# Row means of a Fourier and two-layer kernel: one product per row on four column parts of the array

## The chip, the cores and the metric

One core of a Trainium2 chip. The metric is the device time of one execution in microseconds (us). The engines of the core are TensorE (PE in the profile, PEld its weight loads), VectorE (DVE), ScalarE (ACT), GpSimd (POOL) and SyncE (SP), which only issues transfers here. Transfers run on 16 DMA engines shared by all queues: SP's queue is the hardware queue (q1), GpSimd's accumulating transfers go through the software queue (q0).

## What is computed

```
X = fft(fft(x, axis=1), axis=2).real            # x: 2 x 3008 x 256
rms = sqrt(mean(X * X, axis=-1) + 1e-6)         # one mean per token, 6016 tokens
xn = X / rms * rms_g
h1 = silu(xn @ w_gate) * (xn @ w_val)           # 256 -> 1536
y1 = h1 @ w_out                                 # 1536 -> 256
h = y1 @ w_in                                   # 256 -> 2048
out = (h * cos(h)) @ w_out2                     # 2048 -> 256
```

The result is real and symmetric, so only half of the columns of the spectrum are made, and two mirrored tokens share one column.

## The kernel before

The first stage makes the spectrum. The sequence is split in 32 x 94; after a first transform `features(G)` and `sequence(G)` on TensorE make 34 rows of the grid (`G` = 0 to 33, 17 for each of the 2 batches), 94 columns each, in a loop over `G`. VectorE's `pq_copy` and ScalarE's `uv_copy` (two rows at a time, `p = G // 2`) move the results on, into `uv0` and `uv1`. In the same loop ScalarE, VectorE and GpSimd split the first weights (`w1`, `wo1`) into a high and a low part. The low parts of `w1` and `wo1` are completed by accumulating transfers that GpSimd issues (`w1_add`, `wo1_add`).

The means of squares go over partitions, so TensorE makes them. The 34 rows are cut into 9 parts of 3 to 5 rows (`PARTS`). For part `q`: ScalarE squares (`square`), GpSimd adds the two halves (`add_squares`), TensorE multiplies by one column of weights (`rms`, all rows of the part in one product of 282 to 470 columns into one PSUM partition), ScalarE copies this to `mean_row` (`mean_copy`, two buffers, so part `q` waits for `mean_in[q - 2]`), and SP spreads it to one partition per row (`spread_mean`). `RMS_AT` gives the `G` behind which the product of a part stands on TensorE, `MEAN_COPY_AT` the `p` of the copy. `root`, `recip` and `inverse` make 1 / rms from them, first for the six rows that the first tile needs, and SP stores it and loads it back over all partitions (`store_inv`, `load_inv`).

The second stage takes 6 tiles of 502 columns. In a tile `up1` makes gate and value for 12 chunks of 128, `down` multiplies them into the output of the first layer, two chunks behind; then `up2` and `down` do the same for 16 chunks of the second layer. Every product is done as three (`L518` to `L520`: high by high, high by low, low by high). Of each chunk VectorE forms gate and value, ScalarE takes Silu, GpSimd multiplies, ScalarE and VectorE or GpSimd make `h_hi` and `h_lo`.

Each engine runs its own instructions in the order in which they are written; semaphores tie them together. The queue of SP is written out by hand: in it stand, behind the loads of the inputs, the spreads of the nine parts, the stores of `uv0` and `uv1` to memory, the tile loads and the weight loads `wo1` (1.5 MB), `wo2` and `win2` (2 MB each, `wo_raw` and `win_raw` in the profile). `win2` is asked for when all six chunks of `w1_lo` have landed. In chunk 6 of the first tile ScalarE waits for `win2` and the last chunk of `wo1_lo` (`win2_part`). Two of the nine parts are late: their products stand in the first tile (`RMS_LATE`).

Of the kernel before, what the change touches and what calls it, by code (L numbers as in the profile page):

```python
# [37 lines left out]
MEANS = sum(len(p) for p in PARTS)  # L38
MAGIC = 1.5 * 2.0 ** 23
# [3 lines left out]
def tables():  # L43
# [5 lines left out]
    for b in range(2 * BATCH):  # L49
# [17 lines left out]
    const = np.zeros((P, 2))  # L67
    const[:, 0] = 2.0 / DIM
    const[0, 0] = 1.0 / DIM
    const[1:, 1] = 1.0  # L70
    f = lambda v, c: np.ascontiguousarray(v.reshape(v.shape[0], c), dtype=np.float32)
    return {"t_seq1": f(seq1, 2 * BATCH * 2 * K1), "t_feat": f(feat, FEAT + DIM),
            "t_seq2": f(seq2, K1 * N2), "t_const": f(const, 2)}


def build(nc, x, w1a, w1b, small, wo1, win2, wo2, t_seq1, t_feat, t_seq2, t_const, out):
    ctx = ExitStack()
    with ctx:
# [45 lines left out]
        mean_row = sb("mean_row", [ROWS, MEAN_COLS], o_i2h + WO1B)[0:1, :, :]  # L124
        assert 8 * SQUARES * MEAN_COLS <= WO2B and WO1B + 4 * ROWS * MEAN_COLS <= WI2B
# [30 lines left out]
        consts = sb("consts", [2], o_end + 2016)  # L156
# [5 lines left out]
        assert base + pad(o_end + 2304 + 16 * N2) + 4 * N <= 229344  # L162
        mean_w, mask = consts[:, 0:1], consts[:, 1:2]
# [67 lines left out]
        RMS_AT = [8, 9, 15, 21, 24, 28, 32]  # L231
        MEAN_COPY_AT = [2, 3, 7, 10, 11, 13, 15]
        RMS_LATE = range(len(RMS_AT), MEANS)

        def rms_bank(q):
            return 3 if q < len(RMS_AT) else 6 + q - len(RMS_AT)

# [22 lines left out]
        WO1_SPLIT_AT = {14: 0}  # L260
# [43 lines left out]
        def _(sp):  # L304
# [126 lines left out]
        def _(pe):  # L431
# [63 lines left out]
            def rms(q):  # L495

                a, z = part_cols(q)
# [76 lines left out]
            def tile(t, first=False):  # L574
# [13 lines left out]
                for i in range(2, C1):  # L588
                    up1(t, i, halves=(0,))
                    if first and i == 2:  # L590
                        rms(RMS_LATE[1])
                    up1(t, i, halves=(1,))
                    if first and i == 2:
                        pe.wait_ge(uv_main, LAST)
                        down(t, 0, tokens=(0,))
                        pe.wait_ge(mean_out, MEANS)
# [24 lines left out]
        def _(act):  # L621
# [40 lines left out]
            def square(q):  # L662
                a, z = part_cols(q)
                act.wait_ge(uv_main, part_end(q) + 1)
                if q >= SQUARES:
                    act.wait_ge(ms_done, q - SQUARES + 1)
# [5 lines left out]
            def mean_copy(q):  # L672
                a, z = part_cols(q)
                act.wait_ge(ms_done, q + 1)
                if q >= ROWS:
                    act.wait_ge(mean_in[q - ROWS], 16)
                nc.scalar.activation(mean_row[:, q % ROWS, 0:z - a], ps[0:1, rms_bank(q), 0:z - a],  # L677
                                     ACT.Copy, bias=EPS).then_inc(mean_out, 1)

            def root(group):  # L680
                rows = STAT_ROWS[group]
                for q in STAT_MEANS[group]:
                    act.wait_ge(mean_in[q], 16)
# [35 lines left out]
            for p in range(LAST // 2):  # L719
# [3 lines left out]
                if p == 13:  # L723
# [6 lines left out]
                split_step(p)  # L730

# [34 lines left out]
            def tile(t, first=False, last=False):  # L766
                for i in range(C1):
# [483 lines left out]
```

## Time and profile before

| | |
|---|---|
| Median of 3 runs | 987.53 us (987.35 to 987.87) |
| Profiled execution | 989.1 us |
| Its span | 987.1 us |
| Busy: TensorE, VectorE, ScalarE, GpSimd | 976.0, 743.3, 640.9, 349.5 us |
| First product of the second stage | 62.63 us |

The span is the part of the profiled execution that the instruction trace covers; times below are counted from its start. An idle time in brackets is that of the engine just before the row, with what ended it.

### The profile page before, as it was taken

How to read it: one execution, taken by the hardware profiler on the slowest of the kernel's cores; microseconds unless marked ns; L12 is line 12 of the kernel's file. 1: busy time of each engine (PE TensorE's matmuls, PEld its weight loads, DVE VectorE, ACT ScalarE, POOL GpSimd, SP SyncE). 2: the span in 40 equal slices, each digit the busy share in tenths (PEclk: the TensorE clock that was granted, in tenths of full speed). 3: DMA queues.
4: the chain of work that ended last, by engine and by line, in shares of the span. 5: the costliest groups of instructions: out<-in, count | busy, mean ns of one | idle time of the engine just before them, and what ended most of it. 6: DMA issues, size and time to landing. Idle time of an engine off the chain costs nothing.

```text
span 987.1 us, 12908 instructions
## 1 busy us (share of the span) xinstructions
PE 976.0 (99%) x4468; PEld 808.4 (82%) x4468; DVE 743.3 (75%) x1028; ACT 640.9 (65%) x801; POOL 349.5 (35%) x292
## 2 busy tenths in 40 slices
PE   8989999999999999999999999999999999999998
PEld 8868788888888888888888888888888888888886
DVE  6779878768877668877768887767887767887665
ACT  5578778774468775358775348776447876437777
POOL 0359776017640007650006751005761003771000
PEclk9999999999999999999999999999999999999999
DMA  9689202001010001010001010001000000100001
GB/s 328 170 202 258 61 1 53 1 1 43 1 42 2 0 1 42 0 32 10 0 0 42 0 32 11 0 0 42 0 29 3 0 0 0 42 0 0 0 0 42
DMA packets 14079, 36.77 MB, mean 37 GB/s; under 512 B 2616, under 2 KB 6680, under 8 KB 13656
## 3 DMA queue, kind: packets, MB, share of 16 engines
q1 hardware_dynamic: 11976, 31.62, 9.4%
q0 software_dynamic: 2064, 4.72, 2.7%
q8 instruction: 14, 0.23, 0.1%
q14 instruction: 25, 0.20, 0.1%
HBM read 22.33 MB, written 9.26 MB: 32 GB/s over the span
## 4 chain that ended last, share of the span: by engine, by line
PE 93%; DMA 2%; POOL 2%; DVE 2%; ACT 1%; issue 0%; SPq 0%; ACTq 0%; DVEq 0%
PE ps L518 30%; PE ps L519 30%; PE ps L520 30%; PE ps L474 2%; POOL work L1158 1%; DMA x_sb<-x 1%; DMA wo_lo<-wo_raw 1%; PE ps L492 1%; PE ps L490 1%; PE ps L504 1%; POOL h_lo L1069 0%; SPq L306 0%; DVE x_sb L857 0%; PE ps L460 0%; DVE uv_lo L906 0%
## 5 line engine op out<-in xcount | busy, mean ns | idle before, releaser
L518 PE MATMUL ps<-h_hi,wo_hi 128*128 128x502 f32 x672 | 261.5, 389 | 0.0
L520 PE MATMUL ps<-h_hi,wo_lo 128*128 128x502 f32 x672 | 261.5, 389 | 0.0
L519 PE MATMUL ps<-h_lo,wo_hi 128*128 128x502 f32 x672 | 261.4, 389 | 0.0
L1069 POOL TENSOR_TENSOR h_lo<-work,h_hi 128x502 fp32r<-128x502 f32 x92 | 101.8, 1114 | 372.9 <-ACT h_hi L753 369.9
L738 ACT ACTIVATE h_hi<-work 128x502 fp32r<-128x502 f32 x132 | 82.6, 626 | 173.9 <-POOL work L1158 173.8
L1056 DVE SCALAR_TENSOR_TENSOR work<-work,ps 128x1004 f32<-128x1004 f32 (+1 forms) x109 | 117.2, 1075 | 95.1 <-ACT work L835 94.7
L1042 DVE SCALAR_TENSOR_TENSOR work<-work,ps 128x1004 f32<-128x1004 f32 (+1 forms) x109 | 116.5, 1074 | 48.6 <-ACT work L821 48.5
L518 PE MATMUL ps<-x_hi,win_hi 128*128 128x502 f32 x384 | 150.0, 391 | 0.0
L519 PE MATMUL ps<-x_lo,win_hi 128*128 128x502 f32 x384 | 149.3, 389 | 0.0
L520 PE MATMUL ps<-x_hi,win_lo 128*128 128x502 f32 x384 | 149.2, 389 | 0.0
L518 PEld LDWEIGHTS ps<-h_hi,wo_hi 128*128 128x128 f32 x672 | 126.3, 188 | 26.7 <-DVE h_lo L959 0.6
L520 PEld LDWEIGHTS ps<-h_hi,wo_lo 128*128 128x128 f32 x672 | 126.3, 188 | 25.9
L519 PEld LDWEIGHTS ps<-h_lo,wo_hi 128*128 128x128 f32 x672 | 126.3, 188 | 25.7
L966 DVE SCALAR_TENSOR_TENSOR plus<-u,w,ps 128x502 f32<-128x502 f32 x144 | 105.8, 735 | 52.4 <-PE ps L520 51.7
L821 ACT ACTIVATE work<-ps 128x1004 f32<-128x1004 f32 (+1 forms) x109 | 98.2, 906 | 60.7 <-PE ps L520 59.9
L830 ACT ACTIVATE work<-work 128x1004 f32<-128x1004 f32 (+1 forms) x109 | 102.8, 943 | 31.1 <-DVE work L1042 30.3
L1158 POOL TENSOR_TENSOR work<-work,uv_t 128x502 f32<-128x502 f32 x72 | 99.1, 1399 | 47.0 <-DVE uv_t L975 45.0
L959 DVE TENSOR_TENSOR h_lo<-work,h_hi 128x502 fp32r<-128x502 f32 x172 | 114.2, 702 | 1.3
L518 PE MATMUL ps<-uv_hi,w_hi 128*128 128x502 f32 x288 | 112.7, 391 | 2.3 <-ACT mean_row L677 1.4
L520 PE MATMUL ps<-uv_hi,w_lo 128*128 128x502 f32 x288 | 111.9, 389 | 0.0
L519 PE MATMUL ps<-uv_lo,w_hi 128*128 128x502 f32 x288 | 111.9, 389 | 0.0
L753 ACT ACTIVATE h_hi<-work 128x1004 fp32r<-128x1004 f32 (+1 forms) x109 | 101.7, 938 | 14.6 <-PE ps L520 8.7
(87 smaller groups left out, 1282.0 us busy)
## 6 DMA issues: line engine op xcount, KB each, us to landing
out<-y_sb SPq DMA_DIRECT2D x10, 502.0 KB, 3.2
x_sb<-x SPq DMA_DIRECT2D x6, 768.0 KB, 10.8
w_lo<-w_f POOLq DMA_DIRECT2D x6, 512.0 KB, 7.6
uv_t<-uv_dram SPq DMA_DIRECT2D x6, 502.0 KB, 3.6
wo_raw<-wo SPq DMA_DIRECT2D x1, 2048.0 KB, 8.8
win_raw<-win SPq DMA_DIRECT2D x1, 2048.0 KB, 10.0
raw_b<-w1b SPq DMA_DIRECT2D x3, 512.0 KB, 12.8
raw_a<-w1a SPq DMA_DIRECT2D x3, 512.0 KB, 13.1
```

The lines of the kernel that those rows point to most:

```text
L518: nc.tensor.matmul(acc, w_hi, v_hi, start=start, stop=False)
L519: nc.tensor.matmul(acc, w_hi, v_lo, start=False, stop=False)
L520: return nc.tensor.matmul(acc, w_lo, v_hi, start=False, stop=stop)
L753: nc.scalar.activation(h_hi[j % 2][:, gs, 0:N], work[j % 4][:, gs, :], ACT.Copy).then_inc(hi_done, gs.stop - gs.start)
L821: nc.scalar.activation(work[j % 4][:, gs, :], ps[:, bank_pair(j) + gs.start:bank_pair(j) + gs.stop, 0:N], ACT.Copy, bias=MAGIC).then_inc(r ...
L830: nc.scalar.activation(work[j % 4][:, gs, :], work[j % 4][:, gs, :], ACT.Sin, scale=TURN / 2).then_inc(sin_done, gs.stop - gs.start)
L959: nc.vector.tensor_tensor(h_lo[j % 2][:, g, 0:N], work[j % 4][:, g, :], h_hi[j % 2][:, g, 0:N].bitcast(F32), ALU.subtract).then_inc(hid_sp ...
L966: nc.vector.scalar_tensor_tensor(out=plus[m][:, :], in0=u128[:, :], scalar=w128[:, m * C1 + i:m * C1 + i + 1], in1=ps[:, bank_pair(m), 0:N ...
L1042: nc.vector.scalar_tensor_tensor(out=buf, in0=buf, scalar=MAGIC, in1=pair, op0=ALU.subtract, op1=ALU.subtract).then_inc(frac_done, gs.stop ...
L1056: nc.vector.scalar_tensor_tensor(out=buf, in0=buf, scalar=1.0, in1=pair, op0=ALU.subtract, op1=ALU.mult).then_inc(cos_done, gs.stop - gs.s ...
L1069: nc.gpsimd.tensor_tensor(dst, src, hi.bitcast(F32), ALU.subtract).then_inc(s, 1)
L1158: nc.gpsimd.tensor_tensor(work[i % 3][:, g, :], work[i % 3][:, g, :], value[i % 2][:, g, :], ALU.mult).then_inc(h_done[g], 1)
```

## The change

Of a mean part each row gets a product of its own of 94 columns, with 32 equal columns of weights (`QUARTER` is 32), so that row `i` comes out on PSUM partitions 32 (i mod 4) to 32 (i mod 4) + 31; the fifth row of the last part goes to a second piece of columns ("round"). The constant grows from 2 to 33 columns. The copy then takes 94 columns of up to 128 partitions, and the spread reads one partition out of each 32. Besides this the order is changed in several places: product 3 and copy 3 one step earlier; the split of the scaled tile one step earlier; the last product and copy (part 8) from chunk 2 to chunk 3 of the first tile, in another bank; the copy of part 6 ahead of the first `wo1` split; on SP `store_inv` ahead of `load_tile`, `load_u128` behind `load_inv`, and the `wo1` load ahead of the spread of part 3; on GpSimd some sums moved; and one short Silu on ScalarE behind the first stage.

```
-    const = np.zeros((P, 2))
-    const[:, 0] = 2.0 / DIM
+    const = np.zeros((P, QUARTER + 1))
+    const[:, 0:QUARTER] = 2.0 / DIM
...
-        RMS_AT = [8, 9, 15, 21, 24, 28, 32]
-        MEAN_COPY_AT = [2, 3, 7, 10, 11, 13, 15]
+        RMS_AT = [8, 9, 15, 20, 24, 28, 32]
+        MEAN_COPY_AT = [2, 3, 7, 9, 11, 13, 15]
+        LAST_MEAN_AT = 3
...
-        WO1_SPLIT_AT = {14: 0}
+        WO1_SPLIT_AT = {15: 0}
...
             def spread_mean(q):
-                a, z = part_cols(q)
+                b, k = PART_ROWS[q]
                 sp.wait_ge(mean_out, q + 1)
-                sp.dma_start(stat[stat_rows(*PART_ROWS[q]), 0, :], mean_row[:, q % ROWS, 0:z - a]
-                             ).then_inc(mean_in[q], 16)
+                for r in range(rounds(q)):
+                    n = min(4, k.stop - k.start - 4 * r)
+                    sp.dma_start(stat[stat_rows(b, slice(k.start + 4 * r, k.start + 4 * r + n)), 0, :],
+                                 mean_row[0:QUARTER * (n - 1) + 1:QUARTER, q % ROWS, r * N2:(r + 1) * N2]
+                                 ).then_inc(mean_in[q], 16)
...
-            load_tile(0)
-            load_u128(0)
             sp.wait_ge(inv_done, 1)
             store_inv(0, (slice(0, 1), slice(1, FIRST_ROWS)), 0)
+            load_tile(0)
             sp.wait_ge(inv_out, INV_OUT[0])
             load_inv(0)
+            load_u128(0)
             spread_mean(2)
-            store_uv(0, (slice(FIRST_ROWS, K1 - 1), slice(K1 - 1, K1)))
-            spread_mean(3)
             sp.wait_ge(n1_done, 2 * NG)
             load(wo1_raw[:, :], wo1, wo1_in)
+            spread_mean(3)
+            store_uv(0, (slice(FIRST_ROWS, K1 - 1), slice(K1 - 1, K1)))
             spread_mean(4)
...
-                if q >= len(RMS_AT):
+                if q == RMS_LATE[0]:
                     pe.wait_ge(uv_main, LAST - 2)
-                nc.tensor.matmul(ps[0:1, rms_bank(q), 0:z - a], mean_w, squares[:, q % SQUARES, 0, 0:z - a],
-                                 start=True, stop=True).then_inc(ms_done, 1)
+                if q == RMS_LATE[1]:
+                    pe.wait_ge(plus_done, 2 * LAST_MEAN_AT + 2)
+                for i in range(rows):
+                    r, at = i // 4, i % 4 * QUARTER
+                    nc.tensor.matmul(ps[at:at + QUARTER, rms_bank(q), r * N2:(r + 1) * N2], mean_w,
+                                     squares[:, q % SQUARES, 0, i * N2:(i + 1) * N2], start=True, stop=True
+                                     ).then_inc(ms_done, 1)
...
                     up1(t, i, halves=(0,))
-                    if first and i == 2:
-                        rms(RMS_LATE[1])
+                    if first and i == LAST_MEAN_AT + 1:
+                        pe.wait_ge(mean_out, MEANS)
                     up1(t, i, halves=(1,))
...
+                    if first and i == LAST_MEAN_AT:
+                        rms(RMS_LATE[1])
...
-                if p == 13:
+                if p == 12:
                     split_uv(0)
...
+            act.wait_ge(recip_done, 1)
+            nc.scalar.activation(stat[0:1, 1, 0:1], stat[0:1, 1, 0:1], ACT.Silu)
...
-                        if first and i == 1:
-                            mean_copy(RMS_LATE[1])
...
+                    if first and i == LAST_MEAN_AT:
+                        mean_copy(RMS_LATE[1])
...
-                if G == 31:
+                if G == 30:
                     dve.wait_ge(uv_hi_done, 1)
                     lo_part(uv_lo[:, :, 0:N], uv_t[:, :, :], uv_hi[:, :, 0:N], uv_split)
...
             scale_uv(0)
+            scale_u128(0)
+            w1_add(2)
             add_squares(6)
-            w1_add(2)
-            scale_u128(0)
             w1_add(3)
+            add_squares(7)
             wo1_add(0)
-            add_squares(7)
```

The first place is SP's queue between the inverse of the first six rows and the spread of part 4. `stat<-mean_row` is the spread of a part, here of parts 2 and 3, `wo_raw<-wo 128x3072` the load of `wo1`, `uv_dram<-uv` the store of batch 0. Before:

```order
L363 DMA u_90<-uv_dram 128x502
L343 DMA inv_dram<-stat 1x48 [waits inv_done]
L343 DMA inv_dram<-stat 5x94
L359 DMA inv_t<-inv_dram 128x502 [waits inv_out]
L334 DMA stat<-mean_row 4x1x94 [waits mean_out]
L351 DMA uv_dram<-uv_83 128x2x940 [waits uv_main]
L351 DMA uv_dram<-uv_83 128x2x48
L334 DMA stat<-mean_row 4x1x94 [waits mean_out]
L306 DMA wo_raw<-wo 128x3072 [waits n1_done]
```

And in the changed kernel:

```order
L360 DMA inv_dram<-stat 1x48 [waits inv_done,pq_done,uv_stored]
L360 DMA inv_dram<-stat 5x94
L372 DMA uv_t<-uv_dram 128x2x502
L376 DMA inv_t<-inv_dram 128x502 [waits inv_out]
L380 DMA u_90<-uv_dram 128x502
L350 DMA stat<-mean_row 4x94 [waits mean_out]
L320 DMA wo_raw<-wo 128x3072 [waits n1_done]
L350 DMA stat<-mean_row 4x94 [waits mean_out]
L368 DMA uv_dram<-uv_83 128x2x940 [waits uv_main]
L368 DMA uv_dram<-uv_83 128x2x48
```

The spread of part 3 (the second `stat<-mean_row`) stood ahead of the `wo1` load and now stands behind it.

The second place is ScalarE in the first tile. `work<-work` with `g_ready` is the Silu of a chunk, `mean_row<-ps` the copy of a mean part. Before, from the Silu of chunk 0:

```order
L779 ACTIVATE work_74<-work_74 128x1004 [waits g_ready]
L669 ACTIVATE squares<-uv_84 128x940 [waits ms_done,uv_main]
L677 ACTIVATE mean_row<-ps 1x376 [waits mean_in5,ms_done]
L738 ACTIVATE h_hi_78<-work_74 128x502 [waits h_done1,uv_stored]
L738 ACTIVATE h_hi_78<-work_74 128x502 [waits h_done0]
L677 ACTIVATE mean_row<-ps 1x470 [waits mean_in6,ms_done]
L779 ACTIVATE work_75<-work_75 128x1004 [waits g_ready]
```

In the changed kernel, from the Silu of chunk 3:

```order
L805 ACTIVATE work_74<-work_74 128x1004 [waits g_ready]
L726 ACTIVATE wo_hi<-wo_raw 128x1024
L728 ACTIVATE wo_lo<-wo_hi 128x1024 [waits wo1_hi_done]
L702 ACTIVATE mean_row<-ps 128x94 [waits mean_in6,ms_done]
L702 ACTIVATE mean_row<-ps 32x94
L766 ACTIVATE h_hi_79<-work_74 128x502 [waits h_done1,down_done]
```

The copy of part 8 moved from ahead of the second Silu to behind the fourth and its two split copies. SP issues the 2 MB load of `wo2` behind the spread of this part in both kernels:

```order
L350 DMA stat<-mean_row 4x94 [waits mean_out,uv_stored]
L350 DMA stat<-mean_row 4x94 [waits mean_out] x3
L350 DMA stat<-mean_row 1x2x47
L320 DMA wo_raw<-wo 128x4096 [waits uv_done]
L368 DMA uv_dram<-uv_84 128x2x48 [waits uv_main]
```

This is SP's queue of the changed kernel; before, the row `1x2x47` was part of one transfer of five rows.

## Rows read from the trace of the kernel before

**Rows 1.** The page, part 1: busy time and share of each engine.

```profile
PE 976.0 (99%) x4468; PEld 808.4 (82%) x4468; DVE 743.3 (75%) x1028; ACT 640.9 (65%) x801; POOL 349.5 (35%) x292
```

**Rows 2.** Timeline of TensorE, first stage: start, duration, what.

```profile
40.03 0.61 PE L474 MATMUL ps<-feat,g_sb 128*96 128x129 f32 x4
...
41.70 0.68 PE L474 MATMUL ps<-feat,g_sb 128*96 128x129 f32 x4
...
42.42 0.39 PE L492 MATMUL ps<-seq,pq 96*128 96x94 f32 x2
42.64 0.61 PE L474 MATMUL ps<-feat,g_sb 128*96 128x129 f32 x4
...
43.50 0.61 PE L474 MATMUL ps<-feat,g_sb 128*96 128x129 f32 x4
...
59.78 0.79 PE L504 MATMUL ps<-squares,consts 128*1 128x376 f32 x2
```

**Rows 3.** Timeline of TensorE, its stops and two chunk starts.

```profile
51.68 0.64 PE L504 MATMUL ps<-squares,consts 128*1 128x282 f32 x2 [1.09 <-ACT mean_row L677]
...
62.63 0.47 PE L518 MATMUL ps<-uv_hi,w_hi 128*128 128x502 f32 x1 [0.57 <-DVE uv_lo L906]
...
66.44 0.49 PE L518 MATMUL ps<-uv_hi,w_hi 128*128 128x502 f32 x1 [1.35 <-ACT mean_row L677]
...
73.95 0.95 PE L504 MATMUL ps<-squares,consts 128*1 128x470 f32 x2 [0.79 <-issue]
...
79.02 0.39 PE L518 MATMUL ps<-uv_hi,w_hi 128*128 128x502 f32 x1
...
84.46 0.39 PE L518 MATMUL ps<-uv_hi,w_hi 128*128 128x502 f32 x1
...
114.48 0.49 PE L518 MATMUL ps<-uv_hi,w_hi 128*128 128x502 f32 x1 [0.37 <-DVE uv_t L975]
```

**Rows 4.** Timeline of ScalarE in the first tile, and the chain that ended last.

```profile
74.94 0.55 ACT L677 ACTIVATE mean_row<-ps 1x470 f32<-1x470 f32 x1 [1.40 <-PE ps L504]
...
86.41 1.06 ACT L702 ACTIVATE wo_lo<-wo_hi 128x1024 fp32r<-128x1024 f32 x1
...
105.39 1.16 ACT L707 ACTIVATE win_hi<-win_raw 128x512 fp32r<-128x512 f32 x2 [3.83 <-DMA wo_lo<-wo_raw]
...
94.11 11.20 DMA wo_lo<-wo_raw
```

**Rows 5.** Timeline of SP's queue: issues of the spread of part 2 and two loads.

```profile
49.57 1.13 SPq L334 DMA_DIRECT2D stat<-mean_row  x1
...
76.27 0.43 SPq L306 DMA_DIRECT2D wo_raw<-wo  x1
...
94.06 0.35 SPq L306 DMA_DIRECT2D win_raw<-win  x1
```

**Rows 6.** Transfers by issue, 50 to 56 and 76 to 80 us: size, median us to landing.

```profile
wo_raw<-wo SPq DMA_DIRECT2D x1, 1536.0 KB, 10.2
...
wo_raw<-wo SPq DMA_DIRECT2D x1, 2048.0 KB, 8.8
...
uv_dram<-uv SPq DMA_DIRECT2D x2, 48.0 KB, 12.0
```

**Rows 7.** Stretches: busy time of each engine, granted clock, DMA share, GB/s.

```profile
62.50:66.00 3.50, 2.46 (x14) 2.10 (x14) 2.05 (x5) 2.45 (x4) 0.04 (x1) 1.00 1.11 196
78.00:105.30 27.30, 27.30 (x122) 22.64 (x121) 23.90 (x39) 20.34 (x26) 23.26 (x20) 1.00 0.96 279
79.00:82.00 3.00, 3.00 (x15) 2.48 (x14) 2.84 (x5) 2.82 (x4) 3.00 (x4) 1.00 1.00 410
```

**Rows 8.** Timeline of VectorE's weight mixing and GpSimd's product beside it.

```profile
54.23 1.43 DVE L927 SCALAR_TENSOR_TENSOR w_f<-raw_a,gvec,raw_b 128x512 f32<-128x512 f32 x1
...
53.86 2.73 POOL L1115 TENSOR_TENSOR uv_t<-uv_t,inv_t 128x502 f32<-128x502 f32 x2 [1.67 <-DMA inv_t<-inv_dram]
...
75.34 0.74 DVE L927 SCALAR_TENSOR_TENSOR w_f<-raw_a,sm,raw_b 128x512 f32<-128x512 f32 x1
```

More of the change, by code:

```diff
@@ L38 @@
 MEANS = sum(len(p) for p in PARTS)
+QUARTER = P // 4
 MAGIC = 1.5 * 2.0 ** 23
@@ L123, in build @@
         squares = sb("squares", [SQUARES, 2, MEAN_COLS], o_o2h)
-        mean_row = sb("mean_row", [ROWS, MEAN_COLS], o_i2h + WO1B)[0:1, :, :]
-        assert 8 * SQUARES * MEAN_COLS <= WO2B and WO1B + 4 * ROWS * MEAN_COLS <= WI2B
+        ROUNDS = (max(max(p) for p in PARTS) + 3) // 4
+        mean_row = sb("mean_row", [ROWS, ROUNDS * N2], o_i2h + WO1B)
+        assert 8 * SQUARES * MEAN_COLS <= WO2B and WO1B + 4 * ROWS * ROUNDS * N2 <= WI2B
         feat = sb("feat", [FEAT + DIM], o_o2l)
@@ L161, in build @@
         inv_t = sb("inv_t", [N], pad(o_end + 2304 + 16 * N2))
-        assert base + pad(o_end + 2304 + 16 * N2) + 4 * N <= 229344
-        mean_w, mask = consts[:, 0:1], consts[:, 1:2]
+        o_const = pad(o_end + 2304 + 16 * N2) + pad(4 * N)
+        consts = sb("consts", [QUARTER + 1], o_const)
+        assert base + o_const + 4 * (QUARTER + 1) <= 229344
+        mean_w, mask = consts[:, 0:QUARTER], consts[:, QUARTER:QUARTER + 1]
         ga, gb, g128 = sm[:, 0:1], sm[:, 1:2], sm[:, 2:3]
@@ L229, in part_end, with rounds, mean_rows, quarters @@
             return b * STEPS + k.stop - 1
-        RMS_AT = [8, 9, 15, 21, 24, 28, 32]
-        MEAN_COPY_AT = [2, 3, 7, 10, 11, 13, 15]
+        RMS_AT = [8, 9, 15, 20, 24, 28, 32]
+        MEAN_COPY_AT = [2, 3, 7, 9, 11, 13, 15]
         RMS_LATE = range(len(RMS_AT), MEANS)
+        LAST_MEAN_AT = 3
+        assert len(RMS_LATE) == 2
         def rms_bank(q):
-            return 3 if q < len(RMS_AT) else 6 + q - len(RMS_AT)
+            return 3 if q < len(RMS_AT) else 6 if q < MEANS - 1 else bank_pair(1)
+        def rounds(q):
+            return (PART_ROWS[q][1].stop - PART_ROWS[q][1].start + 3) // 4
+        def mean_rows(q):
+            return sum(k.stop - k.start for _, k in PART_ROWS[:q + 1])
+        def quarters(q):
+            return min(4, PART_ROWS[q][1].stop - PART_ROWS[q][1].start) * QUARTER
         def parts_ending(p):
@@ L495, in rms @@
             def rms(q):
-                a, z = part_cols(q)
+                rows = PART_ROWS[q][1].stop - PART_ROWS[q][1].start
                 pe.wait_ge(const_in, 16)
@@ L595, in tile @@
                         down(t, 0, tokens=(0,))
-                        pe.wait_ge(mean_out, MEANS)
+                        pe.wait_ge(mean_out, MEANS - 1)
                         down(t, 0, tokens=(1,))
@@ L665, in square @@
                 if q >= SQUARES:
-                    act.wait_ge(ms_done, q - SQUARES + 1)
+                    act.wait_ge(ms_done, mean_rows(q - SQUARES))
                 if q == 0:
@@ L672, in mean_copy @@
             def mean_copy(q):
-                a, z = part_cols(q)
-                act.wait_ge(ms_done, q + 1)
+                act.wait_ge(ms_done, mean_rows(q))
                 if q >= ROWS:
-                    act.wait_ge(mean_in[q - ROWS], 16)
-                nc.scalar.activation(mean_row[:, q % ROWS, 0:z - a], ps[0:1, rms_bank(q), 0:z - a],
-                                     ACT.Copy, bias=EPS).then_inc(mean_out, 1)
+                    act.wait_ge(mean_in[q - ROWS], 16 * rounds(q - ROWS))
+                for r in range(rounds(q)):
+                    z = quarters(q) if r == 0 else QUARTER
+                    last = nc.scalar.activation(mean_row[0:z, q % ROWS, r * N2:(r + 1) * N2],
+                                                ps[0:z, rms_bank(q), r * N2:(r + 1) * N2], ACT.Copy, bias=EPS)
+                last.then_inc(mean_out, 1)
             def root(group):
@@ L682, in root @@
                 for q in STAT_MEANS[group]:
-                    act.wait_ge(mean_in[q], 16)
+                    act.wait_ge(mean_in[q], 16 * rounds(q))
                 nc.scalar.activation(stat[rows, 1, :], stat[rows, 0, :], ACT.Sqrt).then_inc(root_done, 1)
@@ L1159, in tile @@
                                                 value[i % 2][:, g, :], ALU.mult).then_inc(h_done[g], 1)
-                    if first and i == 0:
-                        add_squares(MEANS - 1)
                     if i == C1 - 2:
@@ L1164, in tile @@
                     lo1(t, i, 1, hid_ready_first)
+                    if first and i == 0:
+                        add_squares(MEANS - 1)
                     if first and i in W1_SPLIT_LATE:
```

7 lines of the change are left out of this document (3 added, 4 removed).

## Prediction

> **What bounds the kernel now.** I read the page first: TensorE is busy 99% of the span [rows 1], so a stage counts only through the stops of TensorE and through what it computes there. Then I read TensorE in order of time. In the first stage it goes round a loop over 34 columns of the grid, one every 0.86 us (from 42.64 to 43.50), and a mean product makes one step 1.67 (40.03 to 41.70) and the next 0.94 [rows 2]. All stops after the loads lie between 50 and 115 us [rows 3]: 1.09 us at 51.68 for a mean row's copy, 0.57 at 62.63 for `uv_lo`, 1.35 at 66.44 for the seventh mean row, 0.79 at 73.95 for the last mean product, and 0.37 at 114.48. From there no wait of TensorE is listed to the end of the span, and 24 products of 502 columns take 5.44 us (79.02 to 84.46), 0.227 each.
>
> The stop of 0.37 us looks like nothing, but it is the one that decides. ScalarE stands still for 3.83 us until 105.39 for the transfer that `win2_part` waits for, and the chain that ended last goes through that landing: issued 94.11, 11.20 us, landed 105.31 [rows 4]. From there it runs through the copies of `win_hi`, `h_hi` of chunk 6, VectorE's chunk 8 and to TensorE at 114.48. So there is next to no slack behind the landing: if it comes later, TensorE waits later by the same amount, and nothing behind it is idle that could take the loss up. What sets the landing is bandwidth: the 16 DMA engines are busy 0.96 of the 27.3 us from 78.00 to 105.30 [rows 7]. That stretch begins when SP issues the 2 MB load of `wo_raw` at 76.27 [rows 5], and SP issues it behind the spread of the last mean row, which ScalarE finished at 74.94 + 0.55 = 75.49 [rows 4].
>
> **The change part by part.**
>
> *The last mean (part 8).* Before, its product stands in chunk 2 of the first tile, its copy before ScalarE's second Silu. Now the product stands behind `down` of chunk 1 (that is, in chunk 3), and the copy behind Silu and both copies of `split_wo1` in chunk 3. At the old pace chunk 3 ends on TensorE at 84.46 [rows 3]; behind the Silu of chunk 3 the `wo_lo` copy starts at 86.41 and ends 1.06 later, at 87.47 [rows 4]; two copies of 94 columns are estimated at 0.5 together, since one of 470 columns takes 0.55. So at an unchanged pace the last mean row is out at 88.0 instead of 75.49.
>
> SP takes its queue in order: spread of part 8 (now two transfers), `wo_raw` 2 MB, the store of batch 1, `win_raw`. From the mean row to the issue of `wo_raw` SP took 0.78 (75.49 to 76.27); one more issue adds about 0.65. From the issue to the busy stretch it is 1.73 (76.27 to 78.00), and then come 27.3 us of transfers, less what can now run earlier. That is the two accumulations of chunks 4 and 5 into `w_lo`, which hang on GpSimd and not on SP: 1.05 MB, at the 196 GB/s of a stretch with such accumulations [rows 7] 5.3 us. The rest, `wo_raw`, the store, `win_raw` and two accumulations into `wo_lo`, is 22.0 us. The win load itself may be asked for earlier than 94.06 [rows 5], but it queues behind 3.5 MB of the same queue. That a later transfer of one queue doesn't overtake is seen in the 48 KB stores issued behind the 2 MB load: they land after 12.0 us, the load after 8.8 [rows 6].
>
> So the landing is (last mean row) + 0.78 + 0.65 + 1.73 + 22.0 = last mean row + 25.2.
>
> *When the last mean row comes.* Four things move it from 88.0.
> Earlier: the `rms(3)` product and its copy move one step forward, which should remove the 1.09 at 51.68; `store_inv` stands ahead of the two loads, `uv_hi` and `uv_lo` are made one step earlier, which takes away the 0.57; the seventh mean is copied before the split of `wo1`, which takes away the 1.35; and the last mean product with its wait leaves chunk 2 (0.79 and the 0.9 that it takes). Together at most 4.7 us.
> Later, first: the load of `wo1` (1.5 MB) now stands ahead of the spread of part 3. It took 10.2 us to land [rows 6]; issued behind the spread that stood at 49.57 [rows 5], and somewhat sooner, beside an accumulation, it ends near 59 to 61, and the spread of part 3 behind it no sooner. The copy of part 5 reuses that row's buffer (`mean_in3`), and `rms(6)` waits for the copy. TensorE reached that product at 59.78 before [rows 2], and less the 1.09 plus six parts of dearer products it is there at about 59.8 again, so I take a new stop of 1.5 us, between 0 and 2.5 (ScalarE's copy can't be done before 60, and its own start takes time).
> Later, second: the row products. One of 94 columns in this loop takes 0.22 (42.42 to 42.64) [rows 2], four take 0.88. A product of 376 columns adds 0.81 + 0.08 = 0.89 to the loop, its start and end included. The new form isn't in the trace: below, it costs nothing more or saves what two passes overlap; above, 0.3 more per part. I take 0.2, for seven parts 1.4, nearest to the rows of 94 columns.
> Later, third: VectorE and GpSimd. The mixing of weights took 1.43 on VectorE at 54.23, while GpSimd multiplied from 53.86, and 0.74 at 75.34, when GpSimd was idle [rows 8]. Now the second Silu no longer waits for the last mean, so GpSimd's product of chunk 1 falls on the two late mixes. Two of them cost up to 2 x 0.7 us more; I take 1.4 (0 to 1.7), and the up product of chunk 3 waits for VectorE behind them.
> Sum: 88.0 - 4.7 + 1.5 + 1.4 + 1.4 = 87.6; ScalarE is busy in this stretch and takes up part of any difference, so I use 87.3, with 82.5 and 89.5 as ends.
>
> *The release.* 87.3 + 25.2 = 112.5, against 105.3: 7.2 later. TensorE's own work is near its old place there (the four terms cancel within 1 us), so it stops for about 7 us in chunk 8, first at `down` of chunk 6, whose `h_hi` is behind the waiting `win2_part` on ScalarE.
>
> *What costs nothing.* The copies of the other mean rows (fewer columns each than before) lie on ScalarE, which waits elsewhere. The constant of 33 columns instead of 2 is 17 KB under the first loads. The Silu table loaded before the wait (1.3 us) helps only where ScalarE is late in chunk 0; it isn't. Without that cover each would be worth under 1.5 us.
>
> **A page beside the rows.** The row shows 0.22 us for each 94-column product, and nothing of four that overlap [rows 2]. The Trainium skill, "TensorEngine Tiling (Array Packing)", Key Properties, says that tiles of the array run independently and in parallel, and that a change of tiling mode drains the engine. By it four row products would take little more than one, some 0.6 less a part, by the rows 1.4 more in all. The sum to the release hardly moves by this, since the stop for `mean_in3` takes up what TensorE gains before it; the last mean row would come about 1 us sooner.
>
> **The sum.** The profiled execution took 989.1 us for a span of 987.1, the median of the runs is 987.53. Plus 7.2: span 994.3, profiled 996.3, median 994.7.
>
> **The rivals.**
> *Transfers run faster* (ends on the other side). In the stretch from 79 to 82 they moved 410 GB/s, against 279 over the whole [rows 7]. With the accumulations out of the way, the remaining 6.6 MB could go at 410: 16 us instead of 22. With the last mean row at 87.3 the release is at 106.5, 1.2 later: 988.7, no change. If the row comes at 83.3 (all the 4.7 kept) the release is at 102.5 and TensorE keeps up to 2.5: 985.0. The point from which it is a gain is a last mean row before 84. Against it: stretches with stores and accumulations never came near 410, and they make up half of what is left.
> *The first stage gains all and the transfers stay*: 83.3 + 25.2 = 108.5, plus 3.2: 990.7. This is slower too, only smaller.
> *The long stop lowers TensorE's clock.* No row of this trace has TensorE idle for more than 1.5 us after the loads, and the granted clock is 1.00 in every stretch listed [rows 7]; a stop of 7 us is outside what it shows. At half the clock, 1.2 in place of 2.4 GHz, a 502-column product takes about twice its 0.227; over some 12 products that is 2.7 us: 997.4. The Trainium skill, "TensorE: Matmul & The Clock Gate", Part 1, says that an idle engine falls back to 1.2 GHz. This makes the loss larger than the sum.
> *The change does nothing*: if the loads of batch 1 and `wo2` didn't hang on the last mean, the moves inside the first stage would cancel: 987.5. SP's order speaks against it.
>
> **How the numbers follow.** Within 0.2% (985.6 to 989.5) is about what a measurement of this kernel can't tell from no change. The forecast (992 to 996.5) has 0.56, the clock rival (above 996.5) 0.14, the smaller loss (989.5 to 992) 0.14, no change 0.08, faster 0.08. The range from 989 to 999.5 leaves out the faster cases, most of no change, and a stop with a longer clock loss. Slower 0.84, same 0.08, faster 0.08.
>
> **What would show it.** Right: SP issues the 2 MB `wo_raw` load near 88 to 89 us and not 76; the DMA engines stand nearly idle from about 78 to 88; ScalarE's wait for `win_raw` or `wo_lo` is about 8 to 12 us instead of 3.8 and ends near 112; TensorE has one stop of 5 to 8 us near 113 to 119 and none of size behind it; a stop for a mean row near 59 to 61. Wrong: the last mean row out before 84; DMA at over 350 GB/s from its issue on; the landing under 106; or a loss that lies at the means themselves.

## The result, and the profile after

The changed kernel takes 994.54 us (median of 5 runs, 992.32 to 996.86) against 987.87 (5 runs beside it): ratio 1.0059, 95% interval 1.0035 to 1.0084. Forecast: 994.7 (989.0 to 999.5). The profiled execution took 996.86 us, span 995.0 (before 989.1 and 987.1). A second profile, taken later of the same kernel, took 993.09 us, span 991.2; the two differ in one place that matters below, so both are shown.

The page (part 1 answers to [rows 1]; part 6, issues to landing, to [rows 6]):

```profile
PE 978.2 (98%) x4518; PEld 813.3 (82%) x4518; DVE 743.5 (75%) x1028; ACT 639.0 (64%) x803; POOL 351.2 (35%) x292
...
wo_raw<-wo SPq DMA_DIRECT2D x1, 2048.0 KB, 9.6
win_raw<-win SPq DMA_DIRECT2D x1, 2048.0 KB, 19.6
```

The chain over the last mean row: timeline of ScalarE, then of SP's queue, first profile (answers to [rows 4, 5]):

```profile
57.75 0.25 ACT L702 ACTIVATE mean_row<-ps 128x94 f32<-128x94 f32 x1 [1.26 <-DMA stat<-mean_row]
...
87.98 0.35 ACT L702 ACTIVATE mean_row<-ps 128x94 f32<-128x94 f32 x2
...
112.42 1.15 ACT L733 ACTIVATE win_hi<-win_raw 128x512 fp32r<-128x512 f32 x2 [8.20 <-DMA win_raw<-win]
...
89.56 0.40 SPq L320 DMA_DIRECT2D wo_raw<-wo  x1
...
92.81 0.37 SPq L320 DMA_DIRECT2D win_raw<-win  x1
```

The last row is out at 87.98 + 0.35 = 88.33, SP issues the 2 MB load of `wo2` 1.23 us later, and 22.8 us after that `win_raw` has landed and ScalarE goes on. The waiting instruction is the same as before; it ends 7.0 us later.

TensorE, same profile (answers to [rows 2, 3]): two row-product places, the stop at part 6, and the stop at the release with the pace behind it:

```profile
40.22 0.37 PE L525 MATMUL ps<-squares,consts 128*32 128x94 f32 x8
40.52 0.68 PE L491 MATMUL ps<-feat,g_sb 128*96 128x129 f32 x4
...
58.14 0.52 PE L525 MATMUL ps<-squares,consts 128*32 128x94 f32 x8 [1.75 <-ACT mean_row L702]
58.59 1.18 PE L491 MATMUL ps<-feat,g_sb 128*96 128x129 f32 x4
...
88.38 0.49 PE L540 MATMUL ps<-uv_hi,w_hi 128*128 128x502 f32 x1 [1.17 <-ACT mean_row L702]
...
115.82 0.49 PE L540 MATMUL ps<-h_hi,wo_hi 128*128 128x502 f32 x1 [4.04 <-DVE h_lo L979]
...
116.90 0.62 PE L540 MATMUL ps<-h_hi,wo_hi 128*128 128x502 f32 x1
117.32 0.62 PE L541 MATMUL ps<-h_lo,wo_hi 128*128 128x502 f32 x1
```

Stretches of it (columns as in [rows 7]):

```profile
62.50:66.00 3.50, 3.50 (x16) 3.10 (x15) 1.87 (x3) 2.12 (x3) 0.89 (x1) 0.64 0.79 144
70.00:78.00 8.00, 6.23 (x25) 3.91 (x23) 7.97 (x9) 5.44 (x7) 8.00 (x7) 1.00 0.00 0
...
90.00:112.40 22.40, 21.78 (x97) 17.64 (x95) 15.54 (x24) 10.43 (x13) 11.95 (x11) 1.00 0.93 304
...
114.00:118.00 4.00, 2.18 (x6) 1.79 (x7) 3.28 (x4) 4.00 (x7) 3.48 (x3) 0.78 0.01 2
```

The DMA engines stand still from 70 to 78, and from 78 to 88 their share is 0.40; before, the 2 MB load was issued at 76.27 [rows 5]. TensorE's granted clock, 1.00 all through the kernel before, is mixed with the lower level (1.2 GHz) in two places: behind the stop at 58.14 and behind the stop of 4.04 us at 115.82, where products start 0.42 us apart instead of 0.227.

In the second profile only the second drop is there (timelines of TensorE and ScalarE):

```profile
58.04 0.37 PE L525 MATMUL ps<-squares,consts 128*32 128x94 f32 x8 [1.25 <-POOL squares L1124]
...
83.85 0.35 ACT L702 ACTIVATE mean_row<-ps 128x94 f32<-128x94 f32 x2
...
108.08 1.15 ACT L733 ACTIVATE win_hi<-win_raw 128x512 fp32r<-128x512 f32 x2 [7.99 <-DMA win_raw<-win]
...
111.48 0.79 PE L540 MATMUL ps<-h_hi,wo_hi 128*128 128x502 f32 x1 [3.83 <-DVE h_lo L979]
```

The two profiles start the product of part 6 on TensorE within 0.1 us of each other; from there the first falls 4.1 us behind (last row 88.33 against 84.20), and its release, the point at which ScalarE goes on, comes at 112.42 against 108.08. In that stretch lie some 6.5 us at the lower clock, from 58.6 to 65.2.

### The profile page after: what moved, and what is told of

The parts are those of the page before. It is cut to its first block, busy times and chain, and to the rows that moved or that the text cites. A ratio compares the mean times of both kernels' runs of the same rounds, so it can differ in the third digit from the quotient of the medians.

```text
span 995.0 us, 13011 instructions
## 1 busy us (share of the span) xinstructions
PE 978.2 (98%) x4518; PEld 813.3 (82%) x4518; DVE 743.5 (75%) x1028; ACT 639.0 (64%) x803; POOL 351.2 (35%) x292
## 4 chain that ended last, share of the span: by engine, by line
PE 91%; DMA 4%; DVE 2%; SPq 1%; POOL 1%; issue 0%; ACT 0%; DVEq 0%; ACTq 0%; POOLq 0%
PE ps L540 30%; PE ps L542 29%; PE ps L541 29%; DMA win_raw<-win 2%; PE ps L491 1%; DMA x_sb<-x 1%; DMA stat<-mean_row 1%; PE ps L509 1%; PE ps L507 1%; POOL work L1186 0%; SPq L320 0%; DVE plus L994 0%; DVE w_f L955 0%; DVE x_sb L885 0%; PE ps L477 0%
## 5 line engine op out<-in xcount | busy, mean ns | idle before, releaser
L766 ACT ACTIVATE h_hi<-work 128x502 fp32r<-128x502 f32 x132 | 82.5, 626 | 176.9 <-POOL work L1186 176.7
L987 DVE TENSOR_TENSOR h_lo<-work,h_hi 128x502 fp32r<-128x502 f32 x172 | 114.3, 703 | 1.3
```

Of the source, the lines that this page charges most:

```text
L987: nc.vector.tensor_tensor(h_lo[j % 2][:, g, 0:N], work[j % 4][:, g, :], h_hi[j % 2][:, g, 0:N].bitcast(F32), ALU.subtract).then_inc(hid_sp ...
```

## The experiments

**Theory.** The loss is the late last mean row: SP holds the 2 MB load of `wo2` behind its spread, and the landing, ScalarE and TensorE follow. **Rivals.** The loss is made in the first stage (stop for `mean_in3`, slower mixes, low clock there); or the low clock behind the stops is most of it. Eleven edited kernels were run, and the changed kernel again, each beside the kernel before. They ran on three chips (e1 to e5; e6 to e9; e10 to e12 with the changed kernel again), so times from different chips are compared by their ratios to the kernel before. What each profile shows (us; "stop" is TensorE's before `down` of chunk 6):

| kernel | last mean row out | `wo_raw` issue | `win_hi` starts | stop | span | ratio to before (95%) |
|---|---|---|---|---|---|---|
| before | 75.49 | 76.27 | 105.39 | none | 987.1 | 1 |
| changed, first | 88.33 | 89.56 | 112.42 | 4.04 | 995.0 | 1.0059 (1.0035 to 1.0084) |
| after_again | 84.20 | 85.43 | 108.08 | 3.83 | 991.2 | 1.0060 (1.0041 to 1.0080) |
| e1_wo2_first | 85.11 | 67.35 | 100.91 | none | 985.7 | 0.9994 (0.9977 to 1.0011) |
| e2_mean3_first | 86.22 | 87.45 | 110.25 | 3.83 | 992.6 | 1.0042 (1.0028 to 1.0057) |
| e4_before_late_mean | 87.97 | 88.76 | 112.01 | 4.01 | 995.5 | 1.0087 (1.0065 to 1.0110) |
| e5_early_mean | 70.48 | 71.71 | 101.78 | none | 983.6 | 0.9969 (0.9955 to 0.9984) |
| e6_late_mean_filled | 88.34 | 89.12 | 112.33 | 0.35 | 994.1 | 1.0088 (1.0073 to 1.0102) |
| e7_one_product | 87.05 | 87.83 | 110.97 | 3.87 | 993.1 | 1.0085 (1.0072 to 1.0098) |
| e8_early_one_product | 73.17 | 73.96 | 102.84 | none | 984.7 | 0.9987 (0.9978 to 0.9996) |
| e9_early_mean3_first | 70.20 | 71.43 | 102.70 | 0.82 | 984.5 | 0.9980 (0.9966 to 0.9993) |
| e10_packed_only | 72.77 | 74.00 | 104.76 | 0.31 | 986.6 | 0.9994 (0.9981 to 1.0007) |
| e11_squares6_mean3_first | 69.74 | 70.97 | 101.71 | 0.29 | 983.5 | 0.9965 (0.9952 to 0.9979) |
| e12_early_wo2_first | 70.90 | 69.63 | 100.60 | none | 987.3 | 0.9986 (0.9968 to 1.0005) |

**e1_wo2_first.** Only the order of SP is changed: the load no longer stands behind the last spread.

```
-            for q in STAT_MEANS[2]:
+            for q in STAT_MEANS[2][:-1]:
                 spread_mean(q)
             sp.wait_ge(uv_done, LAST)
             load(wo2_raw[:, :], wo2, wo2_in)
             store_uv(1, (slice(0, 1), slice(1, K1 - 1), slice(K1 - 1, K1)))
+            spread_mean(STAT_MEANS[2][-1])
```

> The changed kernel with one edit on SyncE: the 2 MB load of wo2 and the stores of batch 1 are issued ahead of the spread of the last mean row, everything else stays. Theory (the late last mean holds the 2 MB load, and through it the landing that ScalarE's win2_part waits for): the wo_raw issue moves from 89.6 back to 72 to 76 us, the DMA engines are busy from 78 on, the load of win2 starts near 90 on free engines and lands near 102, TensorE's 4.5 us of stops at h_lo near 112 to 116 and the low clock behind them are gone: 986 to 988.5 us. Rival (the loss lies in the means themselves: the stop for mean_in3, the low clock behind it, the slower mixes): 993 to 995 us, with the issue moved all the same.

987.85 us, level with before. The load is issued at 67.35, sooner than the 72 to 76 that I expected. The last mean row is still out only at 85.11, so most of the loss is the load behind it: 0.66% of the time (1.0060 less 0.9994). ScalarE starts `win_hi` with no wait:

```profile
99.95 1.05 ACT L806 ACTIVATE work<-work 128x1004 f32<-128x1004 f32 x1
100.91 1.13 ACT L734 ACTIVATE win_hi<-win_raw 128x512 fp32r<-128x512 f32 x2
```

The rival of the first stage falls. The late mean does cost something by itself: e5, where it is early too, has a span 2.1 us shorter (983.6 against 985.7; the intervals of their ratios overlap). Between 66 and 90 us TensorE's listed stops add up to 4.1 us in e1 and to 2.3 in e5; one of them, 1.19 us at 85.16, is the wait for the last mean row, which the change puts into chunk 4 of TensorE.

**e4_before_late_mean** is the opposite test: the kernel before with only the last mean moved.

```
-            return 3 if q < len(RMS_AT) else 6 + q - len(RMS_AT)
+            return 3 if q < len(RMS_AT) else 6 if q < MEANS - 1 else bank_pair(1)
...
                         down(t, i - 2)
+                    if first and i == 3:
+                        rms(RMS_LATE[1])
...
+                    if first and i == 3:
+                        mean_copy(RMS_LATE[1])
```

> The kernel before with only the last mean moved to where the change has it: product behind down of chunk 1 in chunk 3, in the other bank, copy behind the Silu and the split of wo1 in chunk 3. One product per part, old order of SyncE and of the first stage. Theory (this move alone makes the loss): last mean row out near 87 to 88, wo_raw issued near 88.5, release at 111.5 to 113, no stop for mean_in3: 993.5 to 996 us. Rival (the loss comes from the other edits): within 0.2% of 987.5 us. Second rival (the stop at the release lowers the clock by itself): granted clock under 0.9 in the stretch behind a stop of over 4 us, and 1 to 3 us more, 995.5 to 998.

997.60 us, above the theory's 993.5 to 996 and in the second rival's range: this one edit alone loses more than the whole change, since the change's other edits bring some back. The clock rival's sign is there too: granted clock 0.55 and 0.60 in 114 to 118 and 118 to 122, 13 products at 0.42.

**e5_early_mean** undoes that edit in the changed kernel (product in chunk 2, copy before the second Silu, and with them the bank, the waits and GpSimd's addition of the squares).

```
-                    if first and i == LAST_MEAN_AT:
-                        rms(RMS_LATE[1])
...
+                    if first and i == 2:
+                        rms(RMS_LATE[1])
```

> The changed kernel with only the last mean back in its old place (product in chunk 2, copy before the second Silu, addition of its squares before the lo part of chunk 0); four row products side by side, new order of the transfers and of the first stage stay. Theory: mean row out at 73 to 76 us, wo_raw issued near 75, release at 102 to 105; what is left is the first stage, with its stop for mean_in3 and the lower clock against four stops removed and cheaper row products: 985 to 988 us. Rival (the first stage's own loss counts): 989 to 992 us.

986.05 us, in ratio 0.31% faster than before. Between e5 and the changed kernel lie 0.91% (1.0060 less 0.9969), between before and e4 0.87%: the late mean is worth 8.6 to 9.0 us, all other edits together a gain of about 3.

**e2_mean3_first.** The spread of part 3 back ahead of the load of `wo1`.

```
+            spread_mean(3)
             sp.wait_ge(n1_done, 2 * NG)
             load(wo1_raw[:, :], wo1, wo1_in)
-            spread_mean(3)
```

> The changed kernel with the spread of mean row 3 back ahead of the 1.5 MB load of wo1. Theory: TensorE's stop of 1.75 us at 58.1 is gone and with it the stretch at the lower granted clock (0.64 in 62.5 to 66 us); the first stage ends 4 to 5 us sooner, the last mean row comes 3 to 4 us sooner than 88.3, and since the transfers hang on it the whole kernel gains that: 990 to 992 us. Rival A (ScalarE or the mixes of VectorE, not TensorE, set the time of the last mean row): the row stays at 87 to 88, TensorE waits longer at the release, 993.5 to 995 us. Rival B (the clock did not fall because of the stop): the stop is gone, the granted clock is still near 0.64 somewhere in 58 to 66 us.

993.03 us, above the expected 990 to 992; in ratio 1.0042 against 1.0060, intervals that overlap. ScalarE's wait of 1.26 us is gone, but TensorE still stops 1.27 us at the same product, now for the squares of part 6, and its granted clock is 0.66 in 58 to 62. So `mean_in3` is at most 0.5 us of that stop, and the theory's first half failed: the cause of the stop is that TensorE comes early (see below).

**e7_one_product and e8_early_one_product.** One product and one row per part again, in the changed kernel and in e5's.

```
-                for i in range(rows):
-                    r, at = i // 4, i % 4 * QUARTER
-                    nc.tensor.matmul(ps[at:at + QUARTER, rms_bank(q), r * N2:(r + 1) * N2], mean_w,
-                                     squares[:, q % SQUARES, 0, i * N2:(i + 1) * N2], start=True, stop=True
-                                     ).then_inc(ms_done, 1)
+                nc.tensor.matmul(ps[0:1, rms_bank(q), 0:rows * N2], mean_w[:, 0:1],
+                                 squares[:, q % SQUARES, 0, 0:rows * N2], start=True, stop=True
+                                 ).then_inc(ms_done, 1)
```

> The changed kernel with one product and one row per part again, as before the change (its last mean and all orders stay late and new). Theory (four row products side by side save 0.42 us a part): the first stage is 2 to 3 us longer, the last mean row comes later by up to that, so the release too: 995.5 to 997.5 us, against 994.54 of the changed kernel. Rival (the stops for squares and mean_in3 take up what the products save, so nothing reaches the release): 994 to 995 us.

> The kernel of e5_early_mean (986.05 us) with one product and one row per part again, so that only the orders of the change are left. Theory: the row products' saving of about 0.42 us a part reaches the end when no landing bounds it: 987 to 989 us. Rival (hidden behind stops at the means): 985.5 to 986.5 us.

996.33 and 986.47 us, ratios 1.0085 and 0.9987. The first lies in the theory's range, the second in the rival's. In ratio the row products are worth 0.25% in the one order and 0.18% in the other, about 2 us, and the spans say 1.9 and 1.1 us (993.1 against 991.2, 984.7 against 983.6). Each of the two differences has intervals that overlap, so a gain of 1 to 2 us is likely, not shown. The orders alone (e8) have 0.9987, less than the 0.2% that can be told apart here.

**e10_packed_only.** The row products alone, in the kernel before; all orders are the old ones.

> The kernel before with the row products alone (four side by side, 32 equal weight columns, a row of 94 columns on each part of the array, its copies and small transfers); every order is that of the kernel before, the last mean is in chunk 2. Theory: each part costs TensorE 0.42 us less, 2 to 3 us in all; the last mean row, and with it the 2 MB load and the landing, come 1.5 to 3 us sooner: 985 to 986.3 us, ratio 0.997 to 0.9985. Rival (waits for mean rows, which do not depend on the product, take it up): ratio within 0.999 to 1.001.

Ratio 0.9994: no difference that can be measured; the rival held. TensorE saves time in the loop and gives part of it back at waits there (timeline of TensorE):

```profile
50.71 0.36 PE L523 MATMUL ps<-squares,consts 128*32 128x94 f32 x6 [1.08 <-ACT mean_row L698]
...
58.77 0.37 PE L523 MATMUL ps<-squares,consts 128*32 128x94 f32 x8 [0.34 <-ACT mean_row L698]
62.09 0.46 PE L538 MATMUL ps<-uv_hi,w_hi 128*128 128x502 f32 x1 [1.48 <-DVE uv_lo L928]
```

The wait for `uv_lo` was 0.57 in [rows 3]. More of the gain is lost further on. TensorE starts the last mean product 2.1 us ahead of before (71.87 against 73.95) and chunk 4 1.2 us ahead (83.22 against 84.46), after two stops of 0.35 and 0.39 us for VectorE; the last mean row is out 2.7 us sooner, the release comes only 0.6 us sooner. At the release ScalarE waits, as in the kernel before, for the last accumulation into `wo_lo`, which GpSimd issues and which takes 11.84 us (before 11.20, [rows 4]); chain, then ScalarE:

```profile
92.84 11.84 DMA wo_lo<-wo_raw
...
104.76 1.15 ACT L729 ACTIVATE win_hi<-win_raw 128x512 fp32r<-128x512 f32 x2 [4.44 <-DMA wo_lo<-wo_raw]
```

**e6_late_mean_filled.** e4 with 16 more products, ahead of `down` of chunk 6; they add terms to the sums that don't belong there.

```
+                        if first and i == 8:
+                            for r in range(16):
+                                nc.tensor.matmul(ps[:, 4, 0:N], sum_hi[:, r % 8 * P:(r % 8 + 1) * P],
+                                                 uv_hi[:, 0, 0:N], start=False, stop=False)
                         down(t, i - 2)
```

> The kernel before with the last mean late (as in e4_before_late_mean, which took 997.6 us), and 16 extra products of 502 columns (uv_hi by sum_hi, added into the output sums, so those sums hold terms that don't belong there) ahead of down of chunk 6 in the first tile, where TensorE stood still for 4.01 us. Theory (the low clock behind the stop, 0.42 us a product for 13 products in place of 0.227, comes from TensorE's idling and is paid on top of the stop): TensorE is busy 3.6 of the 4 us, the products behind it run at 0.227 each, granted clock 1.00 in 114 to 122 us; the end comes 2 to 3 us sooner: 994.5 to 996 us. Rival (the clock falls for another reason, such as the burst of work that the release sets off on the other engines): products at 0.42 again, 997 to 998.5 us.

The granted clock stays 1.00, in this profile and as the mean of all 4 runs; e4, with the same release, has 0.996 to 0.998 in all of its 6. Timeline, then stretches, of TensorE:

```profile
111.61 3.79 PE L604 MATMUL ps<-uv_hi,w_hi 128*128 128x502 f32 x16
115.75 0.50 PE L521 MATMUL ps<-h_hi,wo_hi 128*128 128x502 f32 x1 [0.35 <-DVE h_lo L960]
116.08 0.39 PE L522 MATMUL ps<-h_lo,wo_hi 128*128 128x502 f32 x1
...
114.00:118.00 4.00, 3.65 (x17) 2.72 (x16) 3.35 (x4) 3.94 (x7) 3.55 (x3) 1.00 0.01 2
```

So the drop behind the stop comes from TensorE's idling: shown. Its price isn't what I expected. The 13 products are 2.6 us quicker, yet the span is only 1.4 us shorter (994.1 against 995.5; the release came 0.3 later): behind the release TensorE then waits for VectorE (0.39 us at 121.43). That is 1.7 us in the profiles. The ratios, 1.0087 and 1.0088, show no gain at all, but their intervals are wider than 1.7 us.

**e9_early_mean3_first.** e5 with the edit of e2.

> The kernel of e5_early_mean with the spread of mean row 3 back ahead of the load of wo1. Theory: ScalarE no longer waits 0.50 us at 57 for mean_in3, but TensorE's stop of 1.27 us at 57.7 is for the squares of part 6 on GpSimd and stays: 985.5 to 986.5 us, no difference. Rival (the wait on ScalarE matters): 984 to 985.3 us.

984.87 us, ratio 0.9980, where e5 has 0.9969 (0.9955 to 0.9984): no difference that can be told, as the theory had it, though the median by itself lies in the rival's range.

**e11_squares6_mean3_first.** e9 with GpSimd's order changed.

```
+            add_squares(6)
             scale_u128(0)
             w1_add(2)
-            add_squares(6)
```

> The kernel of e9_early_mean3_first (last mean early, mean row 3 ahead of the wo1 load; 984.87 us, of 12 runs 4 with a granted clock of 0.998 or less, three of these at 989 to 990 us) with GpSimd's addition of the squares of part 6 ahead of scale_u128(0) and w1_add(2). Theory: TensorE's stop of 1.25 us at 58 is gone or under 0.5, all runs have a granted clock of 1.00, median 983 to 984.5 us. Rival A (ScalarE's squares, not GpSimd's order, are late): stop stays over 1 us, 984.5 to 986 us. Rival B (the occasional low clock has nothing to do with the stop): stop gone, and still some runs at 0.998 and 988 us or more.

984.40 us, ratio 0.9965: faster than before by 0.35%, the best here, if not distinct from e5. The stop is 1.06 us, so rival A held: GpSimd now waits 1.87 us for the squares from ScalarE before it adds them. The granted clock was 1.00 in all 12 runs. It was below in 16 of 48 runs of the four kernels with a stop of 1.25 to 1.27 us there (e1, e5, e9, e12) and in none of 11 of e8 (stop 0.84). That the stop brings on the drop is not shown. Only the mean clock of those runs is on record, not where it fell, and the stop's length doesn't order the kernels: e10, with stops of 1.08 and 1.48 us in the first stage, has it in 3 of 12 runs, and the kernel before, with 1.09 and 1.35, in 2 of 85.

**e12_early_wo2_first.** e9 with the edit of e1.

> The kernel of e9_early_mean3_first with the 2 MB load of wo2 and the stores of batch 1 issued ahead of the spread of the last mean row. Theory: the wo_raw issue moves from 71.4 to about 67.5 us, ahead of the wo_lo wait that ends at 102.7; the landing comes 2 to 4 us sooner, but TensorE no longer waits for it, so the time is the same: 984.3 to 985.5 us. Rival (the landing still costs): 982 to 984 us.

The load is issued at 69.63, `win_hi` starts at 100.60, and nothing is gained: 987.22 us, ratio 0.9986. The theory's time missed, the rival's more so. Its five fastest runs (983.92 to 984.69) agree with e9; seven others were at 986 to 991, four of them with a granted clock below 1.00, while the profiled one (989.20) had 1.00 and is looked at at the end.

**after_again.**

> The changed kernel again, beside the three others on one chip, with more runs. Both theories: 993.5 to 995.5 us, ratio 1.0055 to 1.0075, a granted clock below 1.00 in every run.

993.95 us, ratio 1.0060, as expected, but one of the 10 runs (991.18) had a clock of 1.00.

**The release and the end.** The table gives one more reading: how far `win_hi` starts from the 105.39 of before, and the span from 987.1. Where TensorE meets the release with a short stop, the two move together: e5 3.6 earlier and 3.5 shorter, e8 2.6 and 2.4, e9 2.7 and 2.6, e10 0.6 and 0.5, e11 3.7 and 3.6, and e6 6.9 later and 7.0 longer. In the five profiles with an unfilled stop of 3.8 us or more the span grows by 0.4 to 1.8 more than the release (e7 5.6 and 6.0, e2 4.9 and 5.5, the changed kernel 7.0 and 7.9, again 2.7 and 4.1, e4 6.6 and 8.4). Those are the profiles with slower products behind it, so this is what the drop costs at the end of a profile. In e1 and e12 TensorE doesn't wait there, and the span doesn't follow (4.5 earlier and 1.4 shorter; 4.8 earlier and 0.2 longer).

## Why the prediction was right, point by point

*The mechanism and the sum.* The mechanism is right, and shown from both sides (e1, e4, e5). That 994.7 meets 994.54 so closely is luck, as the terms below show. The release moved by 7.0 us in the first profile, forecast 7.2, and by 2.7 in the second; in both the landing set it. The SP issue (89.56, forecast 88 to 89), ScalarE's wait (8.20 us, ending at 112.4) and no other stop of size behind it came as said. The transfers did not stand nearly idle to 88, though: from 78 to 88 their share was 0.40.

*From the last mean row to the landing*, the step "last mean row + 25.2". In all six profiles with the load behind a late mean it is 23.9 to 24.1 (88.33 to 112.42, 84.20 to 108.08, 87.97 to 112.01, ...). There the form was right, the term 1.2 too large: the row to the issue took 1.23, not 1.43, and the issue to the landing 22.8, not 23.7. The rival that the 22.0 us would shrink to 16 fell: 304 GB/s over 90 to 112.4. The form doesn't hold for an early mean: in the kernel before, e5 and e8 to e12 the release comes 29.7 to 32.5 us behind the row, and what it waits for is the last accumulation into `wo_lo`, not the load of `win2`. So a row that comes sooner stops paying in full (e10).

*When the last mean row comes* (forecast 87.3, ends 82.5 and 89.5). Here errors cancelled. It was out at 84.20 in the profile without the first low clock, at 88.33 in the other.
- The four stops, 4.7: gone, all four. Smaller stops for VectorE took part of their place (first profile: 2.7 us in six stops from 70.95 to 81.53).
- Row products, "I take 0.2, for seven parts 1.4": this step failed, in sign. Four row products and what follows start 40.22 and 40.52, 0.30 us apart; the step with a mean is 1.25 (39.27 to 40.52) where it was 1.67 [rows 2], so 0.42 less a part, 2.9 in all instead of 1.4 more. I had added the row prices up as if the products could not overlap. The Trainium skill, "TensorEngine Tiling (Array Packing)", Key Properties, has the tiles run in parallel; the 0.30 us for four, against 0.22 for one on the whole array, bear that out, and I gave it too little weight.
- The stop behind the `wo1` load, 1.5: a stop of 1.25 to 1.75 came, but mostly for another reason. The load landed at 57.3, where I had 59 to 61. I put TensorE at that product "at about 59.8 again"; it was there at 56.4, and the squares of part 6, which pass ScalarE and GpSimd, weren't ready before 57.5. Much of the row products' gain is lost here. `mean_in3` adds 0.5 at most (1.75 in the first profile, where ScalarE waits for it, against 1.25 in the second and 1.27 in e2).
- The mixes, 1.4: measured 3.35 us for the two (row below, of the chain of the first profile) against 1.32 before (two of 0.74 that overlap, [rows 8]; the next instruction starts at 76.66): 2.0 more. Right in kind, 0.6 too small.

```profile
74.16 3.35 DVE w_f L955 x2
```

From 88.0: less 4.7, less 2.9, plus 1.25, plus 2.0 is 83.65, against 84.20 measured. In the first profile the low clock brings it to 88.33, near my 87.3; no step had it.

*TensorE's stop*, "about 7 us in chunk 8". It is in chunk 8 at `down` of chunk 6, as said, but 3.8 to 4.0 us long. In the first profile TensorE comes to chunk 8 at 108.90 rather than 106.2 (79.02 and five times 5.44), so part of the 7 us had gone earlier, 1.17 of it in the new wait for the last mean row at 88.38, which no term had; in the second the release itself is only 2.7 later.

*The rivals.* "The long stop lowers TensorE's clock" had 0.14 and should have stood in the sum: in 37 of 38 runs of the kernels with an unfilled stop (the changed kernel both times, e2, e4, e7) the granted clock is below 1.00. Its size, 2.7 for 12 products, is the upper end of the loss at those products (7 to 14 products in the five profiles, 1.4 to 2.7 us), of which 0.4 to 1.8 reaches the end of the profiles. "The first stage gains all" had 0.14 too, with a row at 83.3 and a release at 108.5: the second profile, 84.20 and 108.08, is nearly that case, with the clock's loss on top. So the central number is the median for a reason that I gave only in part: a release 3 to 7 us later, depending on whether the clock falls in the first stage too, plus the drop behind the stop. That an early drop could come at all was in no step, and what brings it on stays open.

*What costs nothing.* The copies, the constant and the early Silu table weren't tried one by one. e8, which keeps the orders, the constant and the early table, is within 0.13% of before.

## What to carry to other kernels

A weight load that stands in a hand-written queue behind a small wait inherits that wait: before moving a product later, look at what the queue holds behind its last consumer, and put the bulk load ahead of it, as e1 does, or leave the product early, as e5 does, which is the faster of the two in the profiles. A cheaper instruction on the busiest engine is worth nothing that can be measured while that engine waits for other things next (e10), and likely a part of its own saving, 1 to 2 of 2.9 us here, once those waits are moved away (e7, e8). When a forecast has a stop of several microseconds on TensorE, its slower products behind it belong in the sum, less what the next wait takes up.

## What the runs showed of the hardware

- Four products of 94 columns (float32), each on 32 columns of the array, take 0.30 us from the start of the first to the next instruction, where one on 128 columns takes 0.22 [rows 2].
- TensorE's granted clock fell to the lower level after stops of 3.8 to 4.0 us and, in two profiles, behind a stop of 1.27 or 1.75 us (e2, the changed kernel's first), though in others not behind one of 1.25 to 1.27. Behind the long stops it came back while TensorE was kept busy, after 7 to 14 products of 502 columns, 3.0 to 5.9 us.
- A small transfer issued behind the 1.5 MB load on the same queue lands no sooner than the load: the spread of part 3, issued at 47.85, landed 9.82 us later (chain of the first profile), the load, issued at 47.36, after 9.9. With the spread ahead of the load (e2) ScalarE doesn't wait for it.

```profile
47.85 9.82 DMA stat<-mean_row
```

- TensorE can be slower with a granted clock of 1.00. In e12's profile products of 502 columns start 0.233 us apart from about 140 to 300 us, in e9's 0.227; that is 87 or 88 records in 20 us instead of 90, and about 4 us. Stretch 200 to 220 of e12, then of e9:

```profile
200.00:220.00 20.00, 20.00 (x87) 16.49 (x86) 12.16 (x15) 14.17 (x14) 3.57 (x4) 1.00 0.00 0
```

```profile
200.00:220.00 20.00, 20.00 (x90) 16.58 (x89) 12.86 (x16) 14.19 (x14) 4.19 (x4) 1.00 0.00 0
```

At chunk 10 of the first tile e12 is 4.0 us ahead of before (114.0 against 118.0), as far as e11 (114.3), and loses it all there. None of the edits touches an instruction of that stretch, and runs 3 to 7 us above a kernel's fastest turn up for the kernel before too (993.94 beside 986.46); their traces aren't on record. What causes it stays open; it is why differences under 0.2% between these kernels are not taken as shown.
